# One transfer per partition half for a block's inputs, gates by tanh, weights in pieces: a recurrent attention and mixture kernel on one core

## The chip, the cores and the metric

The kernel runs on one core of a Trainium2 chip. The metric is the device time of one execution in microseconds (us), the median of several runs. Engines are called by the profile's names: PE is the matrix engine and PEld its weight load, DVE, ACT and POOL are the vector, scalar and GpSimd engines, SP is the engine that issues most transfers. "SPq" is SP's queue of instructions.

## The reference, cut to what matters

Three stages follow one another. The first is a gated linear recurrence over 768 steps for 4 x 8 heads of width 40, the other two are products of its output with expert and dense weights.

```
for t in range(S):                               # 32 heads, S = 768, D = 40
    m_new = maximum(f_gate[t] + m, i_gate[t])
    f_stab, i_stab = exp(f_gate[t] + m - m_new), exp(i_gate[t] - m_new)
    C = f_stab * C + i_stab * outer(v[t], k[t])
    n = f_stab * n + i_stab * k[t]
    y[t] = sigmoid(o_gate[t]) * (C @ q[t]) / maximum(abs(n @ q[t]), 1)
x = y, 3072 tokens x 320
logits = x @ phi; d = softmax over tokens; slots = d.T @ x
slot_out = relu(slots @ w1[e]) @ w2[e]           # 8 experts
x = softmax(logits over slots) @ slot_out
out = ((x @ w_a) * (x @ w_b)) @ w_out
```

## The kernel before, in words

The recurrence is cut into 24 blocks (NB). A unit is 4 heads, there are 8 units (NU), and each unit has 3 blocks (NBLK) of 4 chunks of 64 steps. One pass of the main loop is called iteration n here. PE's order in it is written out by hand: the state updates of block n (`updates`), then the exponents and scores of block n+1, then the two output products of block n (`inner`, `carried`), then from n = 6 on the transposition of block n-6 of the output (`turn`). ACT takes the exponential of block n+1 (L555) and copies a transposed block out of PSUM (`xT_evac`, L545). DVE multiplies scores and exponentials (`weights`), steps the state (`state`, L701) and gathers the output (`gather`). POOL scales the keys (L491) and applies the denominators and the output gate once per unit (`gate`, L480). Everything is in float32 apart from the exponents.

SP issues all transfers, in program order, on one queue. A block's inputs come in five transfers (`load_block`, L369 to L387): keys in both layouts for all 128 partitions (kk, 3 buffers), queries for two times 40 partitions (qT, 4 buffers), values for two times 64 partitions (v, 4 buffers). SP waits before each kind until the block that used the buffer has been read. Twice in this stage SP also issues a whole expert weight of 128 rows x 20480 bytes behind a block (w1, after blocks 8 and 14, L427). The gate inputs og come as four transfers, three of them ahead of block 0, the fourth between blocks 1 and 2 (L407, L417). ACT turns them into gates with its Sigmoid function (`sigmoid`, L531), three at once before the loop and the last when n == 2. `load_exponents` reads back rows that the kernel has written to memory, in runs of 128 bytes for the part called scratch_G.

The last unit's output (blocks 21 to 23) is finished block by block on DVE (`x_last`, L729 to L741). POOL then clears a buffer, PE transposes the remaining blocks, ACT copies all of them, and the logits products begin. After that the order of PE, the weight transfers and all later stages are as the change leaves them, apart from w1[2] and w1[3] in ten transfers instead of two.

Of the kernel before, what the change touches and what calls it, by code (L numbers as in the profile page):

```python
# [47 lines left out]
L = 64  # L48
# [61 lines left out]
def build(nc, qT, kk, v1, og, ig, fg, phi, w1, w2, wab, wo, cst, out):  # L110
    with ExitStack() as ctx:
# [63 lines left out]
        qb = [view(take(4 * CB * L), 4 * CB * L).rearrange("r (p h t) -> r p h t", p=2, h=2) for _ in range(NQ)]  # L175

        KF, KT = 2 * CB * L, 2 * HU * D
        kkb = [view(take(KF + KT), KF + KT) for _ in range(3)]
        kb = [x[:, 0:KF].rearrange("r (p t) -> r p t", p=2) for x in kkb]
        knb = [x[:, KF:KF + KT].rearrange("r (c h e) -> r c h e", c=2, h=HU) for x in kkb]  # L180
        VB = 2 * HU * VW + 8
        vb = [view(take(2 * VB), 2 * VB).rearrange("r (a n) -> r a n", a=2) for _ in range(NQ)]
# [3 lines left out]
        Wb = [view(take(512), 512).rearrange("r (c h t) -> r c h t", c=2, h=HU) for _ in range(2)]  # L186
# [10 lines left out]
        def gview(i, n):  # L197
# [65 lines left out]
        ld_k = [sem(f"ld_k{i}") for i in range(3)]  # L263
        ld_q = [sem(f"ld_q{i}") for i in range(NQ)]
        ld_v = [sem(f"ld_v{i}") for i in range(NQ)]
# [6 lines left out]
            sem(n) for n in ("G_done", "eG_done", "eG_t", "eGt_done", "dm_done", "dcy_ps", "dcy_done", "rows_done"))  # L272
        sig_done, turn_zero, C_zero = sem("sig_done"), sem("turn_zero"), sem("C_zero")
        e_ps, s_ps, u_ps, x_ps, y_ps, t_ps = (sem(n) for n in ("e_ps", "s_ps", "u_ps", "x_ps", "y_ps", "t_ps"))
        e_sb, w_sb, ks_sb, t_sb, x_sb, xT_sb = (
            sem(n) for n in ("e_sb", "w_sb", "ks_sb", "t_sb", "x_sb", "xT_sb"))
        last_sb, c_step, den_done, gate_done = sem("last_sb"), sem("c_step"), sem("den_done"), sem("gate_done")
# [86 lines left out]
        def _(sp):  # L364
# [4 lines left out]
            def load_block(n):  # L369
                u, blk = n // NBLK, n % NBLK  # L370
                t0, tn = blk * CB * L, CB * L
                if n >= 3:
                    sp.wait_ge(s_ps, n - 2)
                    sp.wait_ge(ks_sb, n - 2)
                sp.dma_start(kkb[n % 3], kk[u, blk]).then_inc(ld_k[n % 3], 16)  # L375
                if n >= NQ:
                    sp.wait_ge(x_ps, n - NQ + 1)
                for hp in range(2):
                    rows = slice(64 * hp, 64 * hp + D)
                    sp.dma_start(qb[n % NQ][rows, :, hp, :], qT[u, hp, :, :, t0:t0 + tn]).then_inc(ld_q[n % NQ], 16)  # L380
                if n >= NQ:
                    sp.wait_ge(u_ps, n - NQ + 1)
                    sp.wait_ge(y_ps, n - NQ + 1)
                for par in range(2):

                    sp.dma_start(vb[n % NQ][64 * par:64 * par + 64, par, 0:2 * HU * VW],  # L386
                                 v1[u, 64 * par:64 * par + 64, blk, :]).then_inc(ld_v[n % NQ], 16)  # L387

            def load_exponents(u):
# [11 lines left out]
                for par in range(2):  # L401
                    rows = slice(L + R_B + 3 * par, L + R_B + 3 * par + 3)
                    src = scr_G[:, u * HU:(u + 1) * HU].rearrange("k h (c a t) -> k h c a t", a=2, t=L)
                    sp.dma_start(RE[r][rows], src[:, :, :, par, :]).then_inc(ld_exp[r], 16)  # L404

            for b in range(B - 1):
                sp.dma_start(xtok[:, b], og[b]).then_inc(ld_og[b], 16)  # L407
            sp.wait_ge(zeroed, 4)
            load_block(0)
# [6 lines left out]
            load_block(1)  # L416
            sp.dma_start(xtok[:, B - 1], og[B - 1]).then_inc(ld_og[B - 1], 16)  # L417
            load_block(2)
            load_block(3)
            load_exponents(1)  # L420
            sp.dma_start(phis, phi).then_inc(ld_phi, 16)
# [10 lines left out]
            for i in (2, 3):  # L432
                sp.dma_start(w1s[i], w1[i]).then_inc(ld_w1p[i], 16)
# [21 lines left out]
        def _(pool):  # L455
# [3 lines left out]
            for r in range(NQ):  # L459
                g.memset(vb[r][:].rearrange("r a n -> r (a n)"), 0.0)  # L460
                g.memset(qb[r][:].rearrange("r p h t -> r (p h t)"), 0.0).then_inc(zeroed, 1)
# [5 lines left out]
            for k in range(2):  # L467
                pool.wait_ge(cut_done, k + 1)
                left = g.tensor_tensor([GR, PT[:, 2]][k][:, 0:S], [GB, GR][k][:, 0:S], PT[:, k, 0:S], ALU.subtract)
                left.then_inc([R_done, parts_G][k], 1)  # L470
            pool.wait_ge(parts_G, 1)

            def gate(u):
# [3 lines left out]
                pool.wait_ge(sig_done, b + 1)  # L477
# [5 lines left out]
            for n in range(NB):  # L483
                pool.wait_ge(ld_k[n % 3], 16 * (n // 3 + 1))
# [5 lines left out]
                for c in range(2):  # L490
                    last = g.tensor_tensor(ksb[n % 2][:, c, 0:HU * D].rearrange("r (h e) -> r h e", h=HU), knb[n % 3][:, c],  # L491
# [32 lines left out]
        def _(act):  # L524
            s = nc.scalar
            act.wait_ge(ld_const, 16)
            exponent_rows(s.copy, 0).then_inc(rows_done, 1)

            def sigmoid(b):
                act.wait_ge(ld_og[b], 16)  # L530
# [4 lines left out]
            s.copy(PT[:, 0, 0:S], GB[:, 0:S]).then_inc(cut_done, 1)  # L535
            s.activation(eG, GB[:, 0:S], ACT.Exp).then_inc(eG_done, 1)
            act.wait_ge(R_done, 1)
            s.copy(PT[:, 1, 0:S], GR[:, 0:S]).then_inc(cut_done, 1)
            for b in range(B - 1):
                sigmoid(b)  # L540

            def xT_evac(m):
                u, blk = m // NBLK, m % NBLK
                act.wait_ge(t_ps, m + 1)
                s.copy(xT[:, u % 2, u // 2, CB * blk:CB * blk + CB].rearrange("r c t -> r (c t)"),  # L545
                       turn_ps(m)[:, :]).then_inc(xT_sb, 1)

            for n in range(NB):
                if n == 2:
                    sigmoid(B - 1)  # L550
# [7 lines left out]
            for m in range(NB - 7, NB):  # L558
# [70 lines left out]
        def _(v_):  # L629
# [99 lines left out]
            def x_last(n):  # L729

                chunks = slice(n % NBLK * CB, n % NBLK * CB + CB)
                T, d = Tb[(NU - 1) % 2][:, :, chunks], dnb[(NU - 1) % 2][:, :, :, chunks]
                x = xtok[:, B - 1, chunks, 80:160].rearrange("r c (p d) -> r p c d", p=2)
# [579 lines left out]
```

## Time and profile before

| | us |
|---|---|
| median of 3 runs | 290.74 |
| lowest and highest run | 290.41, 292.62 |
| profiled execution, device time | 292.25 |
| its span, first to last instruction | 290.2 |
| outside the span | 2.05 |
| PE busy in the span | 250.7 (86%) |
| DVE busy | 181.8 (63%) |
| ACT busy | 88.3 (30%) |
| POOL busy | 61.8 (21%) |
| mean rate of all transfers | 189 GB/s, 54.73 MB |

The share of busy time is a mean over stages. The profile divides the span into 40 slices of 7.26 us, in which PE, its granted clock and the transfers can be followed.

### The profile page before, as it was taken

To read this page: it belongs to the slowest core of one execution; us is meant where nothing else is said; L and a number is where in the kernel's file an instruction comes from. 1 tells how busy PE (TensorE), PEld (TensorE's weight loads), DVE (VectorE), ACT (ScalarE), POOL (GpSimd) and SP (SyncE) were. 2 spreads that over 40 slices of the span, in tenths; PEclk is the share of its full clock that TensorE was granted. 3 is DMA by queue.
4 is the path that set the end of the run, shared out by engine and by line. 5 is a ranking of instruction groups with operands and counts; after the bars stand their busy time and mean duration, and the time that the engine had idled before them with its cause. 6 is when DMAs were issued, how large, how long until landed. Compare 5 with 4: busy or idle time off the path is not lost.

```text
span 290.2 us, 7910 instructions
## 1 busy us (share of the span) xinstructions
PE 250.7 (86%) x3264; PEld 208.8 (72%) x3264; DVE 181.8 (63%) x462; ACT 88.3 (30%) x145; POOL 61.8 (21%) x92
## 2 busy tenths in 40 slices
PE   0557698855999499999799998999799999999996
PEld 0546687845999499899657935556656668999995
DVE  6963667842787277888916823355886867555550
ACT  3683511210222113222236002343800003444441
POOL 9502152311325123427030321331000000000000
PEclk9999999995899779999999999999979999999999
DMA  7827866689658965660299999990000000322222
GB/s 247 351 52 252 221 189 196 183 370 262 179 149 323 288 190 153 184 203 2 78 420 419 424 416 381 436 399 24 2 0 0 0 2 0 113 93 90 80 82 90
DMA packets 20131, 54.73 MB, mean 189 GB/s; under 512 B 3744, under 2 KB 14144, under 8 KB 18432
## 3 DMA queue, kind: packets, MB, share of 16 engines
q1 hardware_dynamic: 20096, 54.23, 54.1%
q8 instruction: 26, 0.43, 0.6%
q14 instruction: 9, 0.07, 0.1%
HBM read 49.99 MB, written 4.23 MB: 187 GB/s over the span
## 4 chain that ended last, share of the span: by engine, by line
PE 60%; SPq 12%; DVE 11%; DMA 11%; issue 2%; ACT 2%; DVEq 0%
PE ps L935 52%; DMA attn<-kk 8%; SPq L380 5%; SPq L386 4%; PE ps L1148 3%; PE ps L1026 2%; DVE attn L701 1%; SPq L375 1%; ACT xTreg L545 1%; DMA attn<-scratch_G 1%; DMA scratch_G<-xTreg 1%; PE ps L1154 1%; DMA xTreg<-ig 1%; SPq L404 1%; DVE attn L684 1%
## 5 line engine op out<-in xcount | busy, mean ns | idle before, releaser
L935 PE MATMUL ps<-attn 128*64 128x41 f32 (+3 forms) x2016 | 92.4, 253 | 17.9 <-DMA attn<-kk 10.4
L935 PEld LDWEIGHTS ps<-attn 128*64 128x64 f32 (+1 forms) x2016 | 86.7, 141 | 25.1 <-DMA attn<-kk 10.9
L491 POOL TENSOR_TENSOR attn<-attn 128x160 f32<-128x160 f32 x48 | 21.1, 461 | 86.2 <-issue 54.4
L701 DVE SCALAR_TENSOR_TENSOR attn<-attn,small,ps 128x41 f32<-128x41 f32 x176 | 31.0, 249 | 5.0 <-PE ps L935 5.0
L545 ACT COPY xTreg<-ps 128x512 f32<-128x512 f32 x24 | 13.6, 593 | 63.8 <-PE ps L1026 63.8
L935 PE MATMUL ps<-woreg,tlow 128*128 128x320 f32 x96 | 28.0, 454 | 2.5 <-DVE tlow L885 2.5
L935 PE MATMUL ps<-Whr,Phr 128*128 128x320 f32 x96 | 30.0, 313 | 0.0
L935 PE MATMUL ps<-Whr,Plr 128*128 128x320 f32 x96 | 29.7, 309 | 0.0
L935 PE MATMUL ps<-Wlr,Phr 128*128 128x320 f32 x96 | 29.6, 309 | 0.0
L684 DVE TENSOR_TENSOR attn<-ps,attn 128x512 f32<-128x512 f32 x24 | 16.5, 688 | 19.6 <-issue 13.6
L935 PEld LDWEIGHTS ps<-woreg,tlow 128*128 128x128 f32 x96 | 18.4, 200 | 11.8 <-DVE tlow L885 4.6
L555 ACT ACTIVATE attn<-ps 128x512 f32<-128x512 f32 x24 | 14.3, 597 | 27.3 <-PE ps L935 27.3
L904 DVE TENSOR_TENSOR Plr<-tail,Phr 128x512 fp32r<-128x512 f32 x20 | 13.8, 691 | 13.0 <-ACT Phr L610 13.0
L713 DVE TENSOR_TENSOR attn<-ps,small 128x328 f32<-128x328 f32 x24 | 12.0, 498 | 14.1 <-PE ps L935 14.1
L935 PEld LDWEIGHTS ps<-Whr,Phr 128*128 128x128 f32 x96 | 18.0, 188 | 0.6 <-issue 0.5
L935 PEld LDWEIGHTS ps<-Wlr,Phr 128*128 128x128 f32 x96 | 18.0, 188 | 0.1
L935 PEld LDWEIGHTS ps<-Whr,Plr 128*128 128x128 f32 x96 | 18.0, 188 | 0.0
L587 ACT COPY tail<-ps 128x512 f32<-128x512 f32 x20 | 10.8, 589 | 18.5 <-PE ps L1148 18.5
L318 POOL TENSOR_TENSOR freg<-small 128x512 f32<-128x512 f32 x6 | 8.6, 1429 | 34.6 <-PE ps L1148 22.0
L318 DVE TENSOR_TENSOR freg<-small 128x512 f32<-128x512 f32 x18 | 12.5, 718 | 5.4 <-PE ps L1148 5.4
L1026 PE MATMUL ps<-small,xreg 128*80 128x128 f32 x96 | 14.9, 287 | 0.8 <-ACT xTreg L545 0.8
L610 ACT CAST Phr<-tail 128x512 fp32r<-128x512 f32 x20 | 12.1, 620 | 10.7 <-PE ps L935 10.7
(158 smaller groups left out, 339.8 us busy)
## 6 DMA issues: line engine op xcount, KB each, us to landing
attn<-kk SPq DMA_DIRECT2D x24, 416.0 KB, 4.5
front<-w SPq DMA_DIRECT2D x2, 2560.0 KB, 10.6
tail<-w SPq DMA_DIRECT2D x2, 2560.0 KB, 12.1
xTreg<-w SPq DMA_DIRECT2D x4, 1280.0 KB, 12.9
attn<-v SPq DMA_DIRECT2D x48, 82.0 KB, 3.2
xreg<-og SPq DMA_DIRECT2D x4, 960.0 KB, 7.0
attn<-qT SPq DMA_DIRECT2D x48, 80.0 KB
xreg<-w SPq DMA_DIRECT2D x3, 1280.0 KB, 10.9
```

The lines of the kernel that those rows point to most:

```text
L318: return eng.tensor_tensor(Pt[t % 4], fixed(Ed[:, t], 16), shifted(Ed[:, t], 0, 16), ALU.mult)
L380: sp.dma_start(qb[n % NQ][rows, :, hp, :], qT[u, hp, :, :, t0:t0 + tn]).then_inc(ld_q[n % NQ], 16)
L491: last = g.tensor_tensor(ksb[n % 2][:, c, 0:HU * D].rearrange("r (h e) -> r h e", h=HU), knb[n % 3][:, c], last_col[:, c].unsqueeze(2).to_ ...
L545: s.copy(xT[:, u % 2, u // 2, CB * blk:CB * blk + CB].rearrange("r c t -> r (c t)"), turn_ps(m)[:, :]).then_inc(xT_sb, 1)
L555: s.activation(Eb[n % 2], psE[n % 2][:], ACT.Exp).then_inc(e_sb, 1)
L610: s.copy(Ph[t % 3], Pm[t]).then_inc(one["ph_sb"], 1)
L684: v.tensor_tensor(Wb[n % 2].rearrange("r c h t -> r (c h t)"), psS[n % 2][:], Eb[n % 2], ALU.mult).then_inc(w_sb, 1)
L701: last = v.scalar_tensor_tensor(out=C[:, cc + 1, p], in0=C[:, cc, p], scalar=dcy[:, 2 * u + p, cc:cc + 1], in1=pUv[:, p, c, 0:VW], op0=ALU ...
L713: chain(v.tensor_tensor(T, pXv[:, :, :, 0:VW], eg.unsqueeze(3).to_broadcast([128, 2, CB, VW]), ALU.mult))
L904: v.tensor_tensor(Pl[t % 3], Pm[t], Ph[t % 3].bitcast(F32), ALU.subtract).then_inc(one["pl_sb"], 1)
L935: return t_.matmul(o_, l_, r_, start=start, stop=stop)
L1026: last = t_.transpose(turn_ps(m)[0:80, 128 * c:128 * c + 128], xtok[:, u // 2, blk * CB + c, 80 * (u % 2):80 * (u % 2) + 80], ident)
```

## The change

- A block's inputs are packed on the host into one row per partition. The lower 64 partitions hold queries, values, keys in both layouts; the upper 64 hold keys in both layouts, values, queries. A row has 1672 floats (6688 bytes). SP issues the lower half, ACT the upper half (`load_upper`), each as one transfer of 64 rows. There are 4 buffers for all of it, and a buffer is filled anew once scores, key scaling, updates, inner and carried products of the block four earlier are done.
- The first three blocks are loaded before the gate inputs; the gate inputs og[0] to og[3] come before the loop, before block 4, and behind blocks 6 and 12.
- Gates: 0.5 * tanh(x / 2) + 0.5, as Tanh and then Copy on half an og (one unit) at a time, two units before the loop and one more at n = 4, 7, ...
- w1[0] and w1[1] come in five pieces each of 128 rows x 4096 bytes, one behind each of blocks 4 to 15 except 6 and 12.
- The scratch_G rows are stored with the parities apart, so that they are read in runs of 768 bytes.
- Blocks 21 and 22 of the last unit are gated on POOL. `turn(17)` moves ahead of `carried(23)`, and DVE copies blocks 21 and 23 of the transposed output instead of ACT. The weights buffer Wb moves into memory that was unused in this stage.

```diff
             def load_block(n):
...
-                sp.dma_start(kkb[n % 3], kk[u, blk]).then_inc(ld_k[n % 3], 16)
-                for hp in range(2):
-                    sp.dma_start(qb[n % NQ][rows, :, hp, :], qT[u, hp, :, :, t0:t0 + tn]).then_inc(ld_q[n % NQ], 16)
-                for par in range(2):
-                    sp.dma_start(vb[n % NQ][64 * par:64 * par + 64, par, 0:2 * HU * VW],
-                                 v1[u, 64 * par:64 * par + 64, blk, :]).then_inc(ld_v[n % NQ], 16)
+                if n >= NQ:
+                    done = n - NQ + 1
+                    sp.wait_ge(s_ps, done)
+                    sp.wait_ge(ks_sb, done)
+                    sp.wait_ge(u_ps, done)
+                    sp.wait_ge(y_ps, done)
+                    sp.wait_ge(x_ps, done)
+                else:
+                    sp.wait_ge(zeroed, n + 1)
+                sp.dma_start(in_b[n % NQ][0:64, 0:HALF], blk_in[u, blk, 0]).then_inc(ld_b[n % NQ], 16)
...
-                if n in (8, 14):
-                    sp.dma_start(w1s[n // 12], w1[n // 12]).then_inc(ld_w1p[n // 12], 16)
+                if n in (6, 12):
+                    sp.dma_start(xtok[:, n // 6 + 1], og[n // 6 + 1]).then_inc(ld_og[n // 6 + 1], 16)
+                elif 4 <= n < 16:
+                    j = n - 4 - (n > 6) - (n > 12)
+                    cols = slice(j % 5 * F, j % 5 * F + F)
+                    sp.dma_start(w1s[j // 5][:, cols], w1[j // 5, :, cols]).then_inc(ld_w1p[j // 5], 16)
...
+            def load_upper(n):          # ScalarE, same waits as load_block
+                s.dma_start(in_b[n % NQ][64:128, OTHER:OTHER + HALF], blk_in[n // NBLK, n % NBLK, 1]).then_inc(ld_b[n % NQ], 16)
...
-                s.activation(xtok[:, b], xtok[:, b], ACT.Sigmoid).then_inc(sig_done, 1)
+                x = xtok[:, u // 2, :, 80 * (u % 2):80 * (u % 2) + 80]
+                s.activation(x, x, ACT.Tanh, scale=0.5).then_inc(tanh_done, 1)
+                act.wait_ge(tanh_done, u + 1)
+                s.activation(x, x, ACT.Copy, scale=0.5, bias=0.5).then_inc(sig_done, 1)
...
             for n in range(NB):
-                if n == 2:
-                    sigmoid(B - 1)
                 act.wait_ge(e_ps, n + 1)
...
                 s.activation(Eb[n % 2], psE[n % 2][:], ACT.Exp).then_inc(e_sb, 1)
+                if 2 <= n < NB - 2:
+                    load_upper(n + 2)
+                if n >= 4 and n % NBLK == 1 and n // NBLK + 1 < NU:
+                    sigmoid(n // NBLK + 1)
...
             def scores(n):
-                pe.wait_ge(ld_k[n % 3], 16 * (n // 3 + 1))
-                pe.wait_ge(ld_q[n % NQ], 32 * (n // NQ + 1))
+                pe.wait_ge(ld_b[n % NQ], 32 * (n // NQ + 1))
...
                 inner(n)
+                if n == NB - 1:
+                    turn(n - 6)
                 carried(n)
-                if n >= 6:
+                if 6 <= n < NB - 1:
                     turn(n - 6)
```

## Rows read from the trace of the kernel before

**Rows 1.** The page's slices: granted clock, transfer engines, rate.

```profile
PEclk9999999995899779999999999999979999999999
DMA  7827866689658965660299999990000000322222
GB/s 247 351 52 252 221 189 196 183 370 262 179 149 323 288 190 153 184 203 2 78 420 419 424 416 381 436 399 24 2 0 0 0 2 0 113 93 90 80 82 90
```

**Rows 2.** The page's chain that ended last, by line.

```profile
PE ps L935 52%; DMA attn<-kk 8%; SPq L380 5%; SPq L386 4%; PE ps L1148 3%; PE ps L1026 2%; DVE attn L701 1%; SPq L375 1%; ACT xTreg L545 1%; DMA attn<-scratch_G 1%; DMA scratch_G<-xTreg 1%; PE ps L1154 1%; DMA xTreg<-ig 1%; SPq L404 1%; DVE attn L684 1%
```

**Rows 3.** Timeline of PE: start, duration, operation, count, idle before.

```profile
25.20 2.43 PE L935 MATMUL ps<-attn 128*64 128x128 f32 x48 [0.67 <-DMA attn<-qT]
28.49 2.04 PE L935 MATMUL ps<-attn 128*64 128x41 f32 x52 [0.86 <-DVE attn L701]
32.00 3.36 PE L935 MATMUL ps<-attn 128*64 128x128 f32 x80 [1.47 <-issue]
36.20 5.42 PE L935 MATMUL ps<-attn 82*64 82x256 bf16 x120 [0.85 <-DMA attn<-scratch_G]
...
48.95 5.12 PE L935 MATMUL ps<-attn 128*64 128x128 f32 x116 [0.93 <-issue]
...
68.42 4.92 PE L935 MATMUL ps<-attn 128*64 128x128 f32 x64 [6.71 <-DMA attn<-kk]
...
99.70 4.92 PE L935 MATMUL ps<-attn 128*64 128x128 f32 x64 [3.68 <-DMA attn<-kk]
```

**Rows 4.** Timeline of ACT: gates, table loads and three exponentials.

```profile
29.51 1.80 ACT L531 ACTIVATE xreg<-xreg 128x1920 f32<-128x1920 f32 x1 [3.03 <-DMA xreg<-og]
31.33 1.28 ACT L555 ACT_TABLE_LOAD   x1
...
57.70 0.60 ACT L555 ACTIVATE attn<-ps 128x512 f32<-128x512 f32 x1 [0.46 <-PE ps L935]
...
110.63 0.60 ACT L555 ACTIVATE attn<-ps 128x512 f32<-128x512 f32 x1 [0.45 <-PE ps L935]
...
123.19 0.60 ACT L555 ACTIVATE attn<-ps 128x512 f32<-128x512 f32 x1 [0.46 <-PE ps L935]
```

**Rows 5.** Windows: busy by engine, clock, transfer share, GB/s.

```profile
23.50:57.70 34.20, 27.89 (x632) 25.76 (x630) 23.32 (x83) 9.72 (x13) 10.83 (x20) 1.00 0.71 205
57.70:110.63 52.93, 42.38 (x796) 39.09 (x794) 31.16 (x107) 10.64 (x18) 13.60 (x24) 0.84 0.81 251
110.63:123.19 12.56, 12.40 (x268) 11.49 (x266) 10.31 (x37) 3.55 (x7) 4.54 (x8) 1.00 0.60 159
62.00:66.00 4.00, 0.00 (x0) 0.00 (x0) 0.63 (x4) 0.35 (x1) 0.00 (x0) 0.74 0.96 391
66.00:72.00 6.00, 3.58 (x44) 3.58 (x44) 1.50 (x2) 0.00 (x0) 0.88 (x2) 0.50 1.02 245
70.00:72.00 2.00, 2.00 (x32) 2.00 (x28) 1.50 (x2) 0.00 (x0) 0.00 (x0) 0.50 0.91 226
101.00:103.00 2.00, 2.00 (x30) 2.00 (x28) 1.22 (x2) 0.00 (x0) 0.00 (x0) 0.50 0.94 200
160.00:170.00 10.00, 9.64 (x125) 7.99 (x125) 7.26 (x19) 0.00 (x0) 3.82 (x2) 1.00 1.02 423
```

**Rows 6.** The page's transfer issues: count, size, us to landing.

```profile
attn<-kk SPq DMA_DIRECT2D x24, 416.0 KB, 4.5
front<-w SPq DMA_DIRECT2D x2, 2560.0 KB, 10.6
...
attn<-v SPq DMA_DIRECT2D x48, 82.0 KB, 3.2
```

**Rows 7.** Timeline of the end of the block stage.

```profile
140.24 2.04 PE L935 MATMUL ps<-attn 128*64 128x96 f32 x48 [0.70 <-DVE attn L714]
...
144.26 3.04 ACT L545 COPY xTreg<-ps 128x512 f32<-128x512 f32 x6 [0.79 <-PE ps L1026]
...
147.35 5.37 PE L935 MATMUL ps<-xTreg,small 128*32 128x384 f32 x64
```

More of the change, by code:

```diff
@@ L174, in take, with two @@
             return a - n
-        qb = [view(take(4 * CB * L), 4 * CB * L).rearrange("r (p h t) -> r p h t", p=2, h=2) for _ in range(NQ)]
         KF, KT = 2 * CB * L, 2 * HU * D
[L178 to L182, printed above, removed]
+        QF, VF = 2 * CB * L, 2 * HU * VW
+        HALF, OTHER = QF + VF + KF + KT, QF + VF
+        in_b = [view(take(HALF + OTHER), HALF + OTHER) for _ in range(NQ)]
+        def two(x, c0, pairs):
+            return bass.AP(tensor=x.tensor, offset=x.offset + c0, ap=[list(x.ap[0])] + pairs)
+        qb = [two(x, 0, [[CB * L, 2], [HALF + VF, 2], [1, CB * L]]) for x in in_b]
+        vb = [two(x, QF, [[VF + KF + KT, 2], [1, VF + 8]]) for x in in_b]
+        kb = [x[:, OTHER:OTHER + KF].rearrange("r (p t) -> r p t", p=2) for x in in_b]
+        knb = [x[:, OTHER + KF:HALF].rearrange("r (c h e) -> r c h e", c=2, h=HU) for x in in_b]
         LE = [view(take(S // 2), S // 2).bitcast(BF16) for _ in range(2)]
@@ L185, in build @@
               for _ in range(2)]
-        Wb = [view(take(512), 512).rearrange("r (c h t) -> r c h t", c=2, h=HU) for _ in range(2)]
+        Wb = [Ed[:, 8 * i:8 * i + 8].rearrange("r (c h) t -> r c h t", c=2) for i in range(2)]
         Eb = [view(take(512), 512) for _ in range(2)]
@@ L262, in build @@
         ld_w2e = [sem(f"ld_w2e{i}") for i in range(E)]
-        ld_k = [sem(f"ld_k{i}") for i in range(3)]
-        ld_q = [sem(f"ld_q{i}") for i in range(NQ)]
-        ld_v = [sem(f"ld_v{i}") for i in range(NQ)]
+        ld_b = [sem(f"ld_b{i}") for i in range(NQ)]
         ld_exp = [sem(f"ld_exp{i}") for i in range(2)]
@@ L402, in load_exponents @@
                     rows = slice(L + R_B + 3 * par, L + R_B + 3 * par + 3)
[L403 to L409, printed above, removed]
+                    src = scr_G[:, u * HU:(u + 1) * HU].rearrange("k h (a s) -> k h a s", a=2)
+                    sp.dma_start(RE[r][rows].rearrange("r h c t -> r h (c t)"), src[:, :, par, :]).then_inc(ld_exp[r], 16)
+            for n in range(3):
+                load_block(n)
+            sp.dma_start(xtok[:, 0], og[0]).then_inc(ld_og[0], 16)
             sp.wait_ge(parts_b, 1)
@@ L432, in _ @@
             for i in (2, 3):
-                sp.dma_start(w1s[i], w1[i]).then_inc(ld_w1p[i], 16)
+                for j in range(5):
+                    cols = slice(j * F, j * F + F)
+                    sp.dma_start(w1s[i][:, cols], w1[i, :, cols]).then_inc(ld_w1p[i], 16)
             sp.wait_ge(one["logits_ps"], 2)
@@ L459, in _ @@
             for r in range(NQ):
[L460 to L461 removed]
+                g.memset(in_b[r][:, 0:OTHER], 0.0)
+                g.memset(in_b[r][:, HALF:HALF + OTHER], 0.0).then_inc(zeroed, 1)
             for r in range(2):
@@ L465, in _ @@
             pool.wait_ge(C_zero, 2)
[L467 to L470, printed above, removed]
+            pool.wait_ge(cut_done, 1)
+            g.tensor_tensor(by_par(GR[:, 0:S]), by_par(GB[:, 0:S]), halves(0), ALU.subtract).then_inc(R_done, 1)
+            pool.wait_ge(cut_done, 2)
+            g.tensor_tensor(halves(2), by_par(GR[:, 0:S]), halves(1), ALU.subtract).then_inc(parts_G, 1)
             pool.wait_ge(parts_G, 1)
@@ L503, in _ @@
                         last.then_inc(x_sb, 1)
+            for i in range(2):
+                T, d, x = last_unit(NB - NBLK + i)
+                pool.wait_ge(den_done, NU + i)
+                pool.wait_ge(sig_done, NU)
+                for p in range(2):
+                    last = g.tensor_tensor(x[:, p], x[:, p], T[:, p, :, 0:D], ALU.mult)
+                last.then_inc(last_half, 1)
+                pool.wait_ge(last_half, i + 1)
+                for p in range(2):
+                    last = g.tensor_tensor(x[:, p], x[:, p], d[:, 1, p].unsqueeze(2).to_broadcast([128, CB, D]), ALU.mult)
+                last.then_inc(last_sb, 1)
             pool.wait_ge(y_ps, NB)
@@ L555, in _ @@
                 s.activation(Eb[n % 2], psE[n % 2][:], ACT.Exp).then_inc(e_sb, 1)
+                if 2 <= n < NB - 2:
+                    load_upper(n + 2)
+                if n >= 4 and n % NBLK == 1 and n // NBLK + 1 < NU:
+                    sigmoid(n // NBLK + 1)
                 if n >= 7:
                     xT_evac(n - 7)
-            for m in range(NB - 7, NB):
+            for m in (*range(NB - 7, NB - 3), NB - 2):
                 xT_evac(m)
@@ L756, in _ @@
             gather(NB - 1)
+            den_last(NB - 1)
             x_last(NB - 1)
+            for m in (NB - 3, NB - 1):
+                v_.wait_ge(t_ps, m + 1)
+                v.tensor_copy(turned(m), turn_ps(m)[:, :]).then_inc(xT_sv, 1)
             v.memset(ones, 1.0)
```

117 lines of the change are left out of this document (64 added, 53 removed).

## The prediction

> **What bounds the kernel now.** I read the slices first [rows 1]. PE's granted clock is at its upper level (2.4 GHz) except around slices 10 and 14 to 15, and in those places the transfer engines are full. Then the chain of waits [rows 2]: PE's own products are half of it, but transfers of kk hold 8% of the span and SP's issues of block inputs another 10%, so in the block stage the inputs set the pace. The third view is PE's timeline [rows 3]: waits of 6.71 and 3.68 us, each released by a kk transfer that stood behind a whole w1 in the one queue, and both followed by 64 instructions in 4.92 us. Four shorter waits for inputs (0.67, 1.47, 0.85, 0.93) lie before 49 us. The fourth view is the distance of exponentials [rows 4]: from block 17 to block 20 it is 123.19 - 110.63 = 12.56 us for three blocks, 4.19 each, with PE busy 12.40 of them [rows 5]. This is the pace that PE itself sets. From block 8 to 17, nine blocks take 52.93 us instead of 37.7, at a mean clock of 0.84 [rows 5]. After the block stage the order of everything is the same, so a gain or loss up to the logits is carried to the end.
>
> **The whole w1 transfers go.** Nine blocks at PE's own pace are 3 x 12.56 = 37.7 us. 52.93 - 37.7 = 15.2 us is what the two queue-ups cost, their slow clock included. If pieces and blocks fit beside the products, all of it comes back.
>
> **Start.** Blocks 0 to 3 are there before they are used and ACT has no gates to make at n = 2. Before, it waited 3.03 us for og, worked 1.80 and loaded its table in 1.28 [rows 4]; the exponential of block 2 started at 32.6, when PE had only just got its queries, so both causes ended together and both must go. They do. The four waits of PE, 0.67 + 1.47 + 0.85 + 0.93 = 3.9 us [rows 3], are my gain here. The wait of 0.86 for the state (L701) stays: it is the latency of the loop. The low end is 2 us, if one of the waits turns into another of that kind, the high end 4.5.
>
> **End.** DVE's work for block 21 kept the gathering of block 22 back, and PE waited 0.70 [rows 7]; with the two products on POOL only three short operations are left there. ACT had six copies in a row, 3.04 us, ahead of the logits at 147.35; now DVE takes two and turn(17) is earlier. The last block then sets the end: its gathering, denominators and two products on DVE, one turn, one copy. Against 147.35 I get 146.5, thus 0.8 us, between 0.2 and 1.5.
>
> **ACT's added work.** Per block one issue (bounds: nothing, if it hides in ACT's waits, and about 1 us; SP's issues of v take 0.6), per three blocks Tanh and Copy of 960 columns, each about half of the 1.80, so 2.0 us. With exponential 0.6, copy 0.6 and issue 0.6 the fullest iteration has 3.8 of 4.19 us. It hides as long as an issue is under 1 us. Behind a waiting `load_upper(n + 2)` stand the gates, the copy and the next exponential, but what it waits for (block n-2 read in full) is done before PE starts exponents n. Cost: none, at most 0.3 us in each of 6 iterations.
>
> **Transfers: the term that decides.** A block was 426 KB in kk and 332 KB in queries and values. Now it is 2 x 64 x 6688 bytes = 0.856 MB, all of it in transfers that write one half of the partitions. Large transfers over 128 partitions run at 423 GB/s (160 to 170 us) [rows 5] and at 391 while w1 flows (62 to 66). When the queue-up of block transfers behind w1 is worked off, the engines are full as well (1.02), but move only 245 GB/s (66 to 72), 226 and 200 in the last two microseconds of such stretches. So the block traffic, in which 44% of the bytes are half-width, has a ceiling far below 423. The small packets can be a part of that: queries come in runs of 1 KB, and only on 40 partitions, which the new rows end. The half width stays and grows. No row shows a transfer of 6688-byte rows to 64 partitions. The bounds are 185 (under the lowest row, since now everything is half-width) and 423. I take 245, the nearest long row, because the two differences pull opposite ways.
>
> The sum for the stretch in which weights ride along (blocks 4 to 15): 12 x 0.856 = 10.27 MB at 245 GB/s are 41.9 us. Ten pieces of 0.524 MB at 420 are 12.5 us, two og of 0.983 MB 4.7 us, exponent rows about 0.6. That is 59.7 us. The first issue comes when carried(0) ends, at 28.49 plus 32/52 of 2.04 less the 0.67 won, 29.1 us. I add 2.4 us between issue and landing (v takes 3.2 with its moving [rows 6]): block 15 lands at 91.2. PE at its own pace wants it at 57.70 - 3.9 + 7 x 4.19 = 83.1. So PE waits 8.2 us in all, spread over many blocks by about 1 us (as this is under the idle share of 18% of the stretch 23.5 to 57.7, where the clock stays 1.00 [rows 5], I add no clock loss). In general the wait is 10270 / rate - 33.7 us. It is nothing above 305 GB/s, 17.7 us at 200. Blocks 16 to 23 need 0.856 / 0.245 = 3.5 us of 4.19 and hold nobody up.
>
> On the half width there is a rule that speaks against this change. The Trainium skill, "SBUF — State Buffer", section "Door 1: The DMA port swizzle", says that partitions 0 to 63 reach only 8 of 16 write ports, with 196 GB/s measured and 218 as the limit, and under "Can I just issue two DMAs to hit both halves?" that two at once gain only 6%. The trace agrees so far as its full engines at 200 to 245 GB/s go. Estimated from that page, 208 to 231 GB/s make the wait 15.7 to 10.8 us and the time 286 to 281 us.
>
> **Sum.** 15.2 + 3.9 + 0.8 = 19.9 us, less 8.2, is a gain of 11.7 us. The profiled execution (292.25, of which 290.2 are span) would take 280.5. It stands 1.5 us above the median of its runs, so against 290.74 I predict 279.0 us.
>
> **Rivals.**
> 1. The halves carry each other: while SP's ring writes the lower partitions ACT's writes the upper, and the pair moves at 305 GB/s or more. For it: w1 and blocks with 128 rows do reach 391 to 423. Against it: SP issues the lower half when block n-4 is done, ACT the upper half only after an exponential, some 2.3 us later, which is about as long as a half takes alone. The whole 19.9 us come: 270.8 us. Chance 0.27.
> 2. One half at a time, the page's rule as a mechanism of this kernel: the block bytes move at 200 to 226 GB/s as in the last two microseconds of the stretches [rows 5]. At 213 the wait is 14.5, the gain 5.4, the time 285.3 (282 to 289). Chance 0.20.
> 3. Slower than before: the half-width transfers become the bound of the whole block stage. It decides at about 195 GB/s; below that even blocks 16 to 23 want more than 4.19 us. At 185 the wait is 21.8 us and the last eight blocks add 8 x (4.63 - 4.19) = 3.5, against 19.9 won: 296 us. For it: the lowest row is 200 with 128-row kk still in the mix. Against it: rows of 6688 bytes instead of 1024. Chance 0.06.
> 4. The change doesn't do what it says in ACT: the tables are still changed between Tanh and Exp. Two loads of 1.28 us make the fullest iteration 6.4 us, 2.2 too long, six times: 13 us less won, but partly in the same time as the transfer waits; about 287 us. Chance 0.04. No row shows a Tanh. The Trainium skill, "ScalarE: Activation LUTs", section "Table sets: the hidden batching unit", puts tanh and exp in one set, by which the loads around gates would vanish; the trace agrees only in that each change between Sigmoid and Exp has its load.
>
> **How the numbers follow.** The forecast case, 230 to 300 GB/s for the block bytes, has 0.43 and runs from 281 to 271.5 us. The range takes in rival 1 and most of rival 2: 270 to 289 us. Within 1% is 287.8 to 293.6, about what a measurement can tell from no change; the slow part of rival 2 and half of rival 4 fall there, 0.10. Slower is rival 3 with a little for a cost that I don't see, 0.08. Faster is 0.82.
>
> **What would show it.** Steps right: no PE wait over 2 us in the block stage; exponentials 12.56 us apart per three blocks after block 16; transfer share near 1.0 from 30 to 90 us at 260 to 300 GB/s; ACT with one table load before 30 us; PE's first four waits gone; logits 4.2 us after carried(23). If the share in that stretch is under 0.9 and blocks keep 4.19 us throughout, rival 1 is right. If PE waits over 1.5 us for in_b in most blocks, rival 2. My prediction would fail furthest if the start were held up: og[0] and the scratch rows stand behind three half blocks in SP's queue, and at 200 GB/s their bytes end at about 17 us, just when the scratch rows are to be written.

## The result, and the profile after

The changed kernel takes 302.62 us (median of 4 runs, 301.98 to 303.81), the kernel before 290.69 beside it: a ratio of 1.040 (1.034 to 1.046). Where one of a kernel's runs lies more than 1.5% above its fastest, the ratios here leave it out. The prediction said 279.0 us and is wrong in sign. The profiled execution took 302.13 us, 300.3 of them span.

The page of the changed kernel: slices, the chain by line, and the transfer issues (count, size, us to landing).

```profile
PEclk9999997979799798999999999999999999999999
DMA  7976799999999999788039999996000000222222
GB/s 189 251 214 202 163 247 245 224 226 214 227 251 245 225 204 232 178 209 206 20 92 416 423 422 422 447 400 274 0 2 0 0 0 2 90 87 87 87 91 87
...
PE ps L994 53%; DMA attn<-blk_in 17%; DMA xreg<-og 5%; PE ps L1209 3%; PE ps L1084 2%; DVE attn L754 2%; PE ps L1090 1%; POOL attn L480 1%; PE ps L1215 1%; POOL attn L481 1%; DVE attn L766 1%; ACT xreg L584 1%; ACT freg L619 1%; ACT xreg L582 1%; DVE tlow L384 1%
...
attn<-blk_in SPq DMA_DIRECT2D x24, 418.0 KB, 9.9
attn<-blk_in ACTq DMA_DIRECT2D x24, 418.0 KB, 11.4
front<-w SPq DMA_DIRECT2D x10, 512.0 KB, 16.9
...
xreg<-og SPq DMA_DIRECT2D x4, 960.0 KB, 16.5
```

Against [rows 1]: from slice 5 to 15 (counted from 0) the transfer engines are now full in every slice, where before they were full only behind the two w1. Yet no slice of that stretch reaches 260 GB/s; before, the same place had peaks of 370 and 323. Further on, in slices 21 to 26, the same engines move 400 to 447. So here the engines are full at about half the rate. In the chain, block inputs hold 17% (before, kk and SP's issues of block inputs together 18% [rows 2]) and og 5%. A half block lands 10 to 11 us after its issue, a weight piece of 0.524 MB after 17.

Windows of the changed kernel (length, busy us of PE, PEld, DVE, ACT and POOL, granted clock, mean busy share of the 16 transfer engines, GB/s), against [rows 5]. In short windows the share can come out somewhat above 1.

```profile
10.00:20.00 10.00, 6.10 (x61) 5.23 (x62) 8.77 (x13) 1.87 (x3) 3.81 (x2) 1.00 1.01 272
40.00:120.00 80.00, 58.99 (x1102) 53.36 (x1100) 44.74 (x153) 23.07 (x32) 20.91 (x36) 0.90 1.02 230
120.00:150.00 30.00, 29.71 (x624) 27.47 (x625) 23.95 (x83) 10.29 (x16) 12.06 (x20) 0.98 0.65 155
...
129.50:133.00 3.50, 3.35 (x71) 2.97 (x70) 3.36 (x15) 2.59 (x4) 1.39 (x3) 1.00 0.94 231
160.00:200.00 40.00, 38.47 (x415) 25.10 (x404) 18.64 (x42) 10.60 (x20) 8.13 (x6) 1.00 1.02 424
```

For 80 us the share is 1.02 and the rate 230 GB/s. Behind 120 us the weights are in, the share falls to 0.65 and PE is busy for 29.71 of 30. From 129.5 to 133 only halves are moved, and they reach 231 by themselves, at a share of 0.94.

Timeline of PE, the start, some of the nine waits for block inputs (15.3 us together) and the logits, against [rows 3, 7]:

```profile
24.42 2.38 PE L994 MATMUL ps<-attn 82*64 82x256 bf16 x40 [1.51 <-DMA attn<-scratch_G]
...
46.76 1.97 PE L994 MATMUL ps<-attn 128*64 128x128 f32 x16 [2.38 <-DMA attn<-blk_in]
58.85 1.09 PE L994 MATMUL ps<-attn 128*64 128x128 f32 x16 [2.77 <-DMA attn<-blk_in]
...
97.87 1.97 PE L994 MATMUL ps<-attn 128*64 128x128 f32 x16 [2.65 <-DMA attn<-blk_in]
...
158.52 5.37 PE L994 MATMUL ps<-xTreg,small 128*32 128x384 f32 x64 [0.17 <-issue]
```

Timeline of ACT, the table load, the gates, exponentials and an issue, against [rows 4]:

```profile
5.76 1.28 ACT L339 ACT_TABLE_LOAD   x1 [5.76 <-POOL attn L481]
...
21.80 1.00 ACT L582 ACTIVATE xreg<-xreg 128x960 f32<-128x960 f32 x1 [8.64 <-DMA xreg<-og]
22.83 1.00 ACT L584 ACTIVATE xreg<-xreg 128x960 f32<-128x960 f32 x1
...
25.67 1.07 ACT L604 ACTIVATE attn<-ps 128x512 f32<-128x512 f32 x2
31.84 0.60 ACT L604 ACTIVATE attn<-ps 128x512 f32<-128x512 f32 x1 [5.10 <-PE ps L994]
...
64.71 0.60 ACT L604 ACTIVATE attn<-ps 128x512 f32<-128x512 f32 x1 [0.45 <-PE ps L994]
64.87 0.47 ACTq L571 DMA_DIRECT2D attn<-blk_in  x1
...
147.86 0.60 ACT L604 ACTIVATE attn<-ps 128x512 f32<-128x512 f32 x1 [0.45 <-PE ps L994]
```

Exponentials are the milestones. Block 2 has its at 31.84 (32.63 before), block 8 at 64.71 (57.70), block 17 at 122.77 (110.63), block 23 at 147.86 (135.74). So the kernel loses 7.8 us between blocks 2 and 8, another 5.1 up to block 17, and nothing after. Beside the nine waits for block inputs PE has six more, 6.1 us together, for which the profile shows no releaser; the largest is 1.96 at 75.42 us. From the last exponential to the logits it takes 10.66 us where it took 11.61.

### The profile page after: what moved, and what is told of

It is laid out like the page before. It is cut to its first block, busy times and chain, and to the rows that moved or that the text cites. A ratio compares the mean times of both kernels' runs of the same rounds, so it can differ in the third digit from the quotient of the medians.

```text
span 300.3 us, 7904 instructions
## 1 busy us (share of the span) xinstructions
PE 253.4 (84%) x3264; PEld 210.8 (70%) x3264; DVE 181.9 (61%) x460; ACT 91.0 (30%) x151; POOL 64.8 (22%) x100
## 2 busy tenths in 40 slices
DMA packets 13699, 57.08 MB, mean 190 GB/s; under 512 B 1984, under 2 KB 5664, under 8 KB 12512
## 3 DMA queue, kind: packets, MB, share of 16 engines
q10 hardware_dynamic: 1920, 10.27, 14.3%
## 4 chain that ended last, share of the span: by engine, by line
PE 61%; DMA 22%; DVE 8%; issue 3%; ACT 2%; POOL 2%; SPq 0%; ACTq 0%; DVEq 0%; POOLq 0%
PE ps L994 53%; DMA attn<-blk_in 17%; DMA xreg<-og 5%; PE ps L1209 3%; PE ps L1084 2%; DVE attn L754 2%; PE ps L1090 1%; POOL attn L480 1%; PE ps L1215 1%; POOL attn L481 1%; DVE attn L766 1%; ACT xreg L584 1%; ACT freg L619 1%; ACT xreg L582 1%; DVE tlow L384 1%
## 5 line engine op out<-in xcount | busy, mean ns | idle before, releaser
L994 PE MATMUL ps<-attn 128*64 128x41 f32 (+3 forms) x1632 | 81.0, 255 | 25.3 <-DMA attn<-blk_in 15.3
L994 PEld LDWEIGHTS ps<-attn 128*64 128x64 f32 (+1 forms) x1632 | 71.1, 141 | 33.6 <-DMA attn<-blk_in 17.7
L737 DVE TENSOR_TENSOR small<-ps,attn 128x512 f32<-128x512 f32 x24 | 16.6, 691 | 23.5 <-issue 16.2
L597 ACT COPY xTreg<-ps 128x512 f32<-128x512 f32 x22 | 12.7, 587 | 58.3 <-PE ps L1084 58.3
L994 PE MATMUL ps<-woreg,tlow 128*128 128x320 f32 x96 | 26.8, 437 | 2.7 <-DVE tlow L944 2.7
L994 PEld LDWEIGHTS ps<-woreg,tlow 128*128 128x128 f32 x96 | 17.4, 190 | 11.9 <-DVE tlow L944 5.3
L994 PE MATMUL ps<-attn,small 128*64 128x96 f32 x384 | 22.7, 263 | 0.0
L994 PEld LDWEIGHTS ps<-attn,small 128*64 128x64 f32 x384 | 20.5, 149 | 0.1
L640 ACT COPY tail<-ps 128x512 f32<-128x512 f32 x20 | 10.8, 589 | 18.5 <-PE ps L1209 18.5
L1084 PE MATMUL ps<-small,xreg 128*80 128x128 f32 x96 | 15.3, 291 | 0.5 <-DVE xreg L796 0.5
```

The lines of the kernel that those rows point to most:

```text
L597: s.copy(turned(m), turn_ps(m)[:, :]).then_inc(xT_sb, 1)
L640: s.copy(Pm[t], job_ps(t + t // 4)[:]).then_inc(one["p_sb"], 1)
L737: v.tensor_tensor(Wb[n % 2].rearrange("r c h t -> r (c h t)"), psS[n % 2][:], Eb[n % 2], ALU.mult).then_inc(w_sb, 1)
L994: return t_.matmul(o_, l_, r_, start=start, stop=stop)
L1084: last = t_.transpose(turn_ps(m)[0:80, 128 * c:128 * c + 128], xtok[:, u // 2, blk * CB + c, 80 * (u % 2):80 * (u % 2) + 80], ident)
```

## Experiments

One theory and several rivals stood after the result. Theory W: a transfer that writes only partitions 0 to 63 or 64 to 127 moves at half the rate, whatever its queue, and holds back what is in flight beside it (the expectations call this drag). The rivals blame the number of bytes, the two queues, the size of rows, or the weight pieces. Times are medians; where the text gives "a ratio", it is to the kernel before, run beside.

### Full width, more bytes

Both queues send all 128 partitions, half of the columns each; what a partition doesn't need is sent as zeros. A block grows from 0.856 to 1.286 MB.

```diff
-sp.dma_start(in_b[n % NQ][0:64, 0:HALF], blk_in[u, blk, 0])
+sp.dma_start(in_b[n % NQ][:, 0:1256], blk_in[u, blk, 0])
...
-s.dma_start(in_b[n % NQ][64:128, OTHER:OTHER + HALF], blk_in[n // NBLK, n % NBLK, 1])
+s.dma_start(in_b[n % NQ][:, 1256:2512], blk_in[n // NBLK, n % NBLK, 1])
```

> The changed kernel with one edit: both transfers of a block cover all 128 partitions (1256 columns each, one on either queue), the missing halves sent as zeros, so 1.286 MB per block instead of 0.856. Theory W (width: transfers to one half of the partitions move at about half the rate and hold back what runs beside them): the stretch 40 to 120 us moves 380 to 420 GB/s, PE's waits for in_b fall under 2 us in all, the time is 272 to 280 us. Rival B (bytes: the reads or these rows are the limit at 230 GB/s whatever the width): still about 230 GB/s, half again as many bytes, 325 us or more. Rival Q (two queues at once hinder each other): still under 260 GB/s.

278.61 us (278.18 to 280.01), a ratio of 0.959 (0.953 to 0.964) to the kernel before. One window, and from the page the issues of this kernel:

```profile
40.00:120.00 80.00, 72.54 (x1530) 66.11 (x1527) 61.15 (x206) 29.31 (x43) 24.78 (x46) 1.00 0.98 374
```

```profile
attn<-blk_in SPq DMA_DIRECT2D x24, 628.0 KB, 7.8
attn<-blk_in ACTq DMA_DIRECT2D x24, 628.0 KB, 8.4
```

With half as many bytes again per block, a transfer lands 2 to 3 us sooner, the rate goes from 230 to 374 GB/s, and PE waits 7.0 us for block inputs instead of 15.3. The waits without a releaser fall as well, from 6.1 us to 1.1, so most of them seem to hang on the transfers too. Two details were expected better: 380 to 420 GB/s, and waits under 2 us. The clock is 1.00 instead of 0.90, and with it the costliest group of PE takes 75.3 us instead of 81.0. The bytes were not the trouble. That it was the width, and not the shorter rows (5024 bytes), is settled by the run on rows of 20480 bytes below.

### One queue

Both halves are issued by SP, one behind the other, and ACT issues nothing.

```diff
 sp.dma_start(in_b[n % NQ][0:64, 0:HALF], blk_in[u, blk, 0])
+sp.dma_start(in_b[n % NQ][64:128, OTHER:OTHER + HALF], blk_in[u, blk, 1])
```

> The changed kernel with both halves of a block issued by SyncE, none by ScalarE. Theory W: the rate at full engines stays at 220 to 240 GB/s and the time within 1.5% of the changed kernel (298 to 307 us). Rival Q (two queues): the rate rises to 300 GB/s or more and the time falls under 290 us.

302.28 us (2 runs, 300.19 and 304.37), a ratio of 1.038 (1.028 to 1.049).

```profile
40.00:120.00 80.00, 55.19 (x1032) 49.45 (x1029) 41.65 (x140) 19.15 (x28) 18.00 (x32) 0.89 0.99 218
```

The same time as with two queues within the 4 us between these two runs, and nearly the same rate (218 for 230, a little under the expected 220). PE waits 22.7 us for block inputs in the profiled run, for 15.3. That one queue would raise the rate is refuted; a difference of a few us can't be told.

### Half of the block full width

The keys' 832 columns go as one transfer over 128 partitions, queries and values still by halves. The bytes are those of the changed kernel.

```diff
+sp.dma_start(in_b[n % NQ][:, OTHER:HALF], blk_mid[u, blk])
-sp.dma_start(in_b[n % NQ][0:64, 0:HALF], blk_in[u, blk, 0])
+sp.dma_start(in_b[n % NQ][0:64, 0:OTHER], blk_in[u, blk, 0])
```

> The changed kernel with the same bytes, but the 832 columns that both halves share (the keys) go as one transfer over 128 partitions, and only queries and values (840 columns) as one half each: half of the block bytes are half-width instead of all. Theory W: per block 0.43 MB at 420 and 0.43 MB at 215 GB/s, 3.0 us instead of 4.0, so the rate at full engines is 270 to 300 GB/s and the time 282 to 290 us. Rival B: no change, 300 to 304 us.

288.27 us (287.21 to 289.3), a ratio of 0.992 (0.988 to 0.995).

```profile
60.00:80.00 20.00, 16.82 (x346) 14.78 (x343) 13.25 (x45) 6.74 (x10) 5.43 (x12) 1.00 1.03 277
```

With the width changed for half of the block's bytes, 14.3 of the 24.0 us between the changed kernel and the full-width one come. Priced apart, 5.1 MB of halves at 220 GB/s and 12.3 MB of full width at 410 would move the 17.5 MB of blocks 4 to 15 at 328 GB/s (17.5 / (23 + 30) us); the window has 277. That is a first sign that a full-width transfer beside half-width ones isn't moved at its own rate. The same sum for the changed kernel, 10.3 MB at 231 and 7.2 MB at 420, gives 284 GB/s; it has 230.

### Rows of 20480 bytes, by place

After the block stage, where nothing else is moved, w1[2] goes in row groups 32 to 95, 0 to 31 and 96 to 127, w1[3] in 0 to 63 and 64 to 127.

```diff
-for i in (2, 3):
-    for j in range(5):
-        sp.dma_start(w1s[i][:, cols], w1[i, :, cols])
+for rows in (slice(32, 96), slice(0, 32), slice(96, 128)):
+    sp.dma_start(w1s[2][rows], w1[2, rows])
+for rows in (slice(0, 64), slice(64, 128)):
+    sp.dma_start(w1s[3][rows], w1[3, rows])
```

> The changed kernel with the two expert weights after the block stage, which have the transfer engines to themselves, cut by partitions: w1[2] as rows 32 to 95, then 0 to 31, then 96 to 127; w1[3] as rows 0 to 63, then 64 to 127, all in rows of 20480 bytes from one queue. Theory W in its form by port (the two sides of partition 64): rows 32 to 95 (1.31 MB) move at 400 GB/s or more in 3.3 us, every other piece at 200 to 220, 3.1 us for each 32 rows and 6.2 us for each 64. Rival N (the number of rows in a transfer counts, not which): rows 32 to 95 are as slow as 0 to 63. Rival B: all at 420. Device time within 1.5% of the changed kernel by all of them.

305.13 us in one run, 0.8% above the changed kernel, as expected. Windows in which rows 32 to 95 are moved (the first two) and the halves of w1[3] (the last two):

```profile
154.00:155.00 1.00, 0.93 (x9) 0.93 (x10) 0.87 (x3) 0.15 (x1) 0.75 (x1) 1.00 1.00 430
155.00:156.00 1.00, 0.83 (x12) 0.45 (x14) 0.83 (x5) 0.00 (x0) 0.96 (x2) 1.00 1.09 471
...
162.00:168.00 6.00, 5.70 (x53) 4.99 (x53) 4.50 (x11) 4.28 (x9) 0.00 (x0) 1.00 0.97 201
168.00:174.00 6.00, 6.00 (x88) 5.78 (x85) 5.44 (x13) 0.00 (x0) 1.26 (x2) 1.00 1.04 218
```

64 rows that lie across the middle move at 430 GB/s and more; 64 rows on one side of it at 201 to 218, and the rows are the longest in this kernel. Over 160 to 174 us the mean is 210 at a share of 1.01. So it is neither the number of rows nor their size, but which side of partition 64 they lie on.

### Two halves at once

w1[2] goes alone; when it has landed, SP issues rows 0 to 63 of w1[3] (163.39 us) and ACT rows 64 to 127 (163.47).

```diff
+sp.dma_start(w1s[2], w1[2])
+sp.wait_ge(ld_w1p[2], 16)
+sp.dma_start(w1s[3][0:64], w1[3, 0:64])
...
+s.dma_start(w1s[3][64:128], w1[3, 64:128])     # ScalarE, after ld_w1p[2]
```

> The changed kernel with w1[2] after the block stage in one transfer over 128 partitions, alone, and then w1[3] as rows 0 to 63 from SyncE and rows 64 to 127 from ScalarE at the same time, each 1.31 MB in rows of 20480 bytes. Theory W in its lockstep form (both queues' packets go through the same engines in turn, and all engines serve one side at a time): w1[2] at about 420 GB/s in 6.2 us, w1[3] at 210 to 240 GB/s in 11 to 12 us. Rival H (the halves carry each other, my rival 1 before): w1[3] also at 350 GB/s or more, 6 to 7.5 us.

```profile
158.00:160.00 2.00, 2.00 (x32) 1.00 (x28) 0.00 (x0) 0.00 (x0) 0.87 (x1) 1.00 0.95 410
...
166.00:168.00 2.00, 2.00 (x18) 1.84 (x17) 1.85 (x5) 1.69 (x3) 0.00 (x0) 1.00 1.04 215
168.00:170.00 2.00, 1.70 (x15) 1.41 (x16) 1.34 (x4) 1.96 (x5) 0.00 (x0) 1.00 0.83 184
170.00:172.00 2.00, 2.00 (x31) 2.00 (x33) 1.97 (x4) 0.61 (x2) 0.34 (x1) 1.00 1.13 256
```

306.39 us in one run. The whole tensor alone moves at 410 GB/s and lands 10.4 us after its issue. Its like in two halves at once moves at 184 to 256, and the halves land after 11.8 (SP's) and 16.8 (ACT's), where 11 to 12 were expected for both. Opposite halves on two queues do not add: rival 1 of the prediction is refuted where it has its best chance. (w2, the second expert weight, stands behind in SP's queue and shares the later part of this stretch.)

### A full-width transfer beside halves

ACT issues the whole of w1[2], 2.62 MB over 128 partitions, and SP the two halves of w1[3] 0.6 us later.

```diff
+s.dma_start(w1s[2], w1[2])                     # ScalarE, after the last copy
...
+sp.dma_start(w1s[3][0:64], w1[3, 0:64])
+sp.dma_start(w1s[3][64:128], w1[3, 64:128])
```

> The changed kernel with w1[2] after the block stage in one transfer of 128 rows from ScalarE's queue and, some 3 us later, w1[3] as rows 0 to 63 and then 64 to 127 from SyncE's, rows of 20480 bytes, so that a full-width and a half-width transfer run side by side. With drag: while both run, all together move 230 to 290 GB/s, and w1[2] lands 10 us or more after its issue, though it needs 6.2 us of transfer alone. Without drag (the full-width one keeps 420 GB/s for its part of the time, as the prediction priced it): the same total, by 2.6 MB at 420 and 2.6 MB at 210, would be 280 GB/s too, so the split is told by the packets' share: w1[2] is done within 8 us of its issue only if it isn't held back.

A window and, from the answer on transfers, the issue on ACT's queue:

```profile
165.00:175.00 10.00, 9.70 (x103) 8.84 (x105) 7.99 (x19) 4.73 (x9) 1.15 (x1) 1.00 1.03 215
```

```profile
tail<-w ACTq DMA_DIRECT2D x1, 2560.0 KB, 22.5
```

312.05 us in one run. The tensor lands after 10.4 us alone (above, from SP's queue) and after 22.5 beside halves (here, from ACT's). Sharing by itself makes it later, so the rate is what tells: priced apart, 2.62 MB at 420 and 2.62 MB at 213 GB/s would take 18.5 us, at 280 GB/s. The window has 215, no more than halves have alone and less than the 230 that were expected at least. So the full-width bytes in flight beside halves move no faster than these. This is the drag on the weight pieces, without the block stage around it. How it comes about no run here shows.

### The pieces in the kernel before

w1[0] and w1[1] in ten pieces behind blocks 4 to 13, all else as before.

```diff
-if n in (8, 14):
-    sp.dma_start(w1s[n // 12], w1[n // 12])
+if 4 <= n < 14:
+    sp.dma_start(w1s[j // 5][:, cols], w1[j // 5, :, cols])
```

> The kernel before with one part of the change alone: w1[0] and w1[1] in ten pieces of 0.524 MB, one behind each of blocks 4 to 13, everything else as before. Theory W with drag (full-width pieces are slowed by the half-width transfers beside them, so all bytes together move at about 250 GB/s): a block and a piece are 1.28 MB, 5.1 us against 4.19, over ten blocks 9 us of waits less the slack of the buffers, against 15.2 lost before: 284 to 289 us. Rival P (the pricing of the prediction, pieces at 420 GB/s and only the block bytes at 245): 4.35 us per block, nearly all of the 15.2 us come back, 276 to 280 us.

284.73 us (282.67 to 285.88), a ratio of 0.980 (0.973 to 0.987), in theory W's range and not in rival P's.

```profile
60.00:80.00 20.00, 18.97 (x402) 17.03 (x398) 14.86 (x51) 5.33 (x10) 6.24 (x11) 1.00 0.92 271
```

Pieces behind the old transfers gain some 6 us. The two stalls (10.4 us) are gone, but where PE had four short waits besides (3.9 us), it now has ten of 0.36 to 2.19 us, 9.9 together; five of them lie before 53 us. This run is a weaker witness for drag than the one before: the engines are busy for 0.92 of the window, not for all of it, and 271 GB/s is above the 250 that theory W named. Some of its waits can have another cause than full engines.

### The changed kernel with whole w1

```diff
-elif 4 <= n < 16:
-    sp.dma_start(w1s[j // 5][:, cols], w1[j // 5, :, cols])
+if n in (8, 14):
+    sp.dma_start(w1s[n // 12], w1[n // 12])
```

> The changed kernel with w1[0] and w1[1] whole behind blocks 8 and 14 again. Theory W with drag: the same bytes go through engines that are full either way, but a whole w1 in the lower half's queue for some us moves partly alone at up to 400 GB/s while PE stands still, so the time is within 3 us of the changed kernel (299 to 306 us). Rival P (pieces as such do the harm, as many small transfers): the time falls under 295 us.

298.28 and 303.28 us in two runs, beside 302.6 with pieces; they are too far apart for a ratio. The window is of the longer one.

```profile
40.00:120.00 80.00, 58.91 (x1100) 53.61 (x1099) 44.44 (x154) 22.08 (x31) 19.16 (x35) 0.87 0.94 232
```

232 GB/s against 230, at a share of 0.94 against 1.02. Both runs are above 295 us, so it isn't the pieces as such that do the harm. Whether whole weights are the same or up to 4 us better these two runs can't tell: the shorter one lies under the expected 299 to 306 and under every run of the changed kernel.

### Gates and end alone

The kernel before with gates by tanh and the new end; transfers, their order and the whole w1 as before. The edit is the L582, `turn` and `last_unit` part of the change.

> The kernel before with the parts of the change that move no transfer: gates by Tanh and Copy one unit at a time, last unit's blocks 21 and 22 on GpSimd, turn(17) ahead of carried(23), two of the last copies on VectorE. Transfers, their sizes and their order as before. By the prediction's sum the end gives 0.8 us and the gates nothing by themselves, since PE waits for its queries at the same place: 289 to 290.5 us, ratio 0.994 to 1.0. If ScalarE's gates were the cause of the early waits, 3 us or more come: under 288 us.

289.2 us (12 runs, 287.37 to 292.29), a ratio of 0.998 (0.995 to 1.001): 0.6 us, about what the end was to bring (0.8), and inside what a measurement can tell from nothing.

### Pieces later, with the old and with the full-width rows

Ten pieces behind blocks 9, 10, 11, 13, 14, 16, 17, 19, 20 and 22, first on the gates-and-end kernel with the old five transfers, then on the full-width kernel. In the two expectations e1 is the full-width kernel, e5 the pieces in the kernel before, e7 gates and end alone, and e6 the second run of this section.

```diff
+PIECES = (9, 10, 11, 13, 14, 16, 17, 19, 20, 22)
-elif 4 <= n < 16:
+elif n in PIECES:
```

> e7 and the ten pieces of w1[0] and w1[1] behind blocks 9, 10, 11, 13, 14, 16, 17, 19, 20 and 22; block inputs in the five transfers of the kernel before, 0.758 MB with 44% of them half-width. Theory W with drag: a block and a piece are 1.28 MB at 250 GB/s, 5.1 us, but four of fourteen blocks have no piece (3.0 us), so 4.5 us on average against 4.19 and the buffers take most of the rest: 278 to 282 us, better than e5 with its ten pieces in a row (284.7), and behind e6 because the early waits stay. If the pieces could be had for their 1.25 us, 275 us.

283.34 us (282.57 to 283.64), a ratio of 0.977 (0.973 to 0.982). The expectation was too low; spreading pieces over places with less traffic gained next to nothing over blocks 4 to 13. PE's waits are 9.1 us; some 5 of them lie before 50 us, ahead of the first piece (issued at 59.28), and the transfer engines are busy for only 0.76 of the stretch 40 to 120 us. So full engines alone don't explain this time; the 1.1 to 1.4 us that PE waits at three of the later blocks have no releaser in the profile and stay open.

> The full-width kernel e1 with the ten pieces spread out, behind blocks 9, 10, 11, 13, 14, 16, 17, 19, 20 and 22 instead of 4 to 15. Theory W: at 410 GB/s a block takes 3.1 us of 4.19 and a piece 1.25, so early blocks no longer wait and later ones seldom do; of the 8 us of waits for block inputs in e1 5 or more go: 271 to 275 us, the fastest of all. If the waits were not from the bytes but from the latency between freeing a buffer and filling it, the time stays at 277 to 279 us.

275.51 us (6 runs, 274.43 to 276.71), a ratio of 0.948 (0.944 to 0.953), just past the expected end. One window, and the largest of the waits for block inputs that are left:

```profile
40.00:120.00 80.00, 76.53 (x1608) 69.42 (x1608) 63.05 (x213) 29.80 (x44) 28.36 (x50) 1.00 0.97 379
```

```profile
46.70 1.09 PE L995 MATMUL ps<-attn 128*64 128x128 f32 x16 [0.88 <-DMA attn<-blk_in]
```

The same pieces in the same places take 283.3 us beside old transfers and 275.5 beside full-width ones. Width isn't the only difference: the order of the first transfers is another, and 4.7 of the 7.8 us are there at the exponential of block 8 (60.28 against 55.55), before pieces can matter. PE now waits 2.0 us for block inputs, so latency from freeing a buffer to filling it was not what kept the full-width kernel at 278.6. This version is some 15 us faster than the kernel before and 27 faster than the changed one, though its transfers move 67.40 MB where the others move 54.73 and 57.08.

## Why the prediction was wrong

**The step that failed: transfers.** The prediction saw that the block bytes had a ceiling near 245 GB/s, but it let the weight pieces and og, 7.2 MB of the 17.5, pass beside them at 420. No row supported that: the 391 GB/s that I read "while w1 flows" came from a stretch in which PE stood still and the block inputs were queued behind w1 [rows 3, 5]. The whole mix moved at 230. With the prediction's own sum, 17.5 MB at 230 GB/s and 0.6 us for the exponent rows are 76.6 us instead of 59.7, and the wait is 29.1 + 76.6 + 2.4 - 83.1 = 25.0 us instead of 8.2. That is 16.8 of the 23.0 us by which block 23's exponential misses its forecast (135.74 - 15.2 - 3.9 + 8.2 = 124.8; measured 147.86), more than the 10 us that the range left above 279. At 245 for everything the wait would already have been 20.3 and the prediction 291: one rate for every byte was enough to lose the gain. The rate of the halves alone wasn't far off, 231 measured for 245. The run with a full-width transfer beside halves shows this drag by itself, and the run with half of the block full width fits it (277 GB/s for 328 priced apart). Of the prediction's own signs, the share near 1.0 came, but at 230 GB/s and up to 120 us instead of 260 to 300 up to 90, and three of PE's waits for block inputs are over 2 us, where none was to be.

**What sets the rate.** The runs show that the side of partition 64 decides, not row length, row count, queue or bytes. The Trainium skill, "SBUF — State Buffer", section "Door 1: The DMA port swizzle", explains it by ports: partitions 0 to 63 reach 8 of 16, 64 to 127 the other 8. By its table rows 32 to 95 reach all 16. The measured 201 to 218 GB/s for halves and 430 to 471 for rows 32 to 95 agree with it; the 231 of the 3.5 us window lies 6% above the 218 that it gives as the limit of 8 ports. The prediction quoted this rule and let it move the wait by 3 to 8 us only, since it applied it to the block bytes alone. That full-width transfers fall to this rate too is told by the runs: 215 GB/s for all that was in flight together.

**Start: predicted a gain of 3.9 us, got 0.8 up to block 2.** The three half blocks stand ahead of og and the scratch rows. og arrives at 21.8 us and ACT sits idle for 8.64 before the gates; the scratch rows land 5.2 to 5.6 us after their issue, where 2.6 were enough before; PE waits 1.51 for them. The first exponential is 2.2 us late (25.67 against 23.49) and block 4's upper half goes out at 32.0, not at 29.1 as assumed, which passes 2.9 us on to a stretch that is bound by transfers. Two of the four waits that it wanted back (1.47 and 0.93) had no releaser in the profile, and it took them for waits on inputs. The prediction named this as the place where it would fail furthest; the larger failure was elsewhere. In the full-width version og is there at 17.44 and the first exponential comes at 23.33.

**Blocks 16 to 23: "hold nobody up".** Blocks 16 and 17 still came late (PE waits 1.23 and 1.94 us), since the backlog of weights wasn't worked off: 13.43 us for two blocks where 8.4 were priced, 5.0 us more. From 17 on it holds: 25.09 us for six blocks, 12.55 for three, as forecast. The three items, 16.8, 2.9 and 5.0, make 24.7 us for 23.0: they explain 1.7 us too much, all of it before block 15, and which of them is too large stays open. The profiled executions differ from forecast by 21.6 us (302.13 against 280.5), since the end and the stages behind it took 1.4 us less than forecast.

**Clock.** I added no loss, as idle was spread. It was 0.90 over 40 to 120 us, against 1.00 at full width. It isn't counted in again above, by the argument that the transfers set the pace there; no run separates the two. What a low clock costs can be seen in the kernel before: the 64 instructions behind each stall took 4.92 us, and 2.67 at a clock of 1.00 with pieces. The prediction's reading of the slices left out a further fall, to 0.7 in slice 29 (counted from 0), behind the block stage with the transfer engines idle; nothing in its sum hangs on it.

**Right.** The stalls of 6.71 and 3.68 us are gone. ACT loads its table once before 30 us, and its issue takes 0.47 us and hides, so rival 4 is out. The end gained 0.95 us from the last exponential to the logits (0.8 predicted), and gates and end alone gained 0.6. That most of the 15.2 us would come back if the transfers fit was right too: at full width, with pieces spread, blocks 8 to 17 take 40.0 us (exponentials at 55.55 and 95.55) instead of 52.9, which is 12.9 us. That whole kernel gains 15 us of the 19.9 that were to be won.

**Not tested alone.** The order of the first transfers, the one wait for all of a block's buffers and the longer exponent rows have no run of their own. They are in the full-width kernels too, which are faster than the kernel before, so they don't cost the 12 us by themselves.

**The rivals.** Rival 1 is refuted by the run of both halves at once. Rival 2 had the right mechanism for the halves, but its price of 285.3 (up to 289) left out the drag in the same way, and its sign came only in part: four waits for block inputs are over 1.5 us, not most blocks. Rival 3 had the right sign for a wrong reason: halves reach 231 GB/s, well above its 195, and blocks alone keep PE's pace. Its price of 296 us was the nearest by luck.

## What to carry to other kernels

Before anything is repacked, look at which partitions a transfer writes: one that stays on one side of partition 64 moved at half rate here, from SP's queue and from SP's and ACT's together, and so did everything in flight beside it. Filling up rows to 128 partitions, with zeros if need be, was worth more than the half as many bytes that it added. Where the profile shows full transfer engines at half the usual rate, price every byte of the stretch at that rate, and don't lend an idle-time rate to the rest.

## What the hardware showed beyond that

A 2.62 MB transfer over 128 partitions needed 10.4 us alone and 22.5 us when 64-row transfers from another queue were in flight, at 215 GB/s for all together, where equal bytes at 420 and 213 would make 280; I had expected the port limit to hold only for the transfer that is narrow. And 1.5 times the bytes arrived sooner: 643 KB over 128 partitions landed in 7.8 us (median, full-width kernel), 428 KB over 64 in 9.9 (changed kernel).
